# Attention: products of the identity in spare columns of two banks, at each step and around the first solve

## The chip, the cores and the metric

The kernel runs on one core of a Trainium2 chip. The metric is the device time of one execution in microseconds; the median of three runs of the kernel before is 908.11 us.

## The reference

Three parts follow each other. The change is in the first, a linear attention with a delta rule; for each of 4 x 8 heads, over 768 tokens and a head dimension of 48:

```python
k_n = k / (np.linalg.norm(k, axis=-1, keepdims=True) + 1e-06)
for t in range(S):
    y[:, :, t] = np.einsum('bhd,bhde->bhe', q[:, :, t], state)
    v_old = np.einsum('bhde,bhd->bhe', state, kt)
    state = state + bt[:, :, :, None] * np.einsum('bhd,bhe->bhde', kt, vt - v_old)
```

Its result goes through a mixer (real part of a two-dimensional Fourier transform, normalisation, two matrix products of width 1536) and a gated layer (products of width 1024 and one over the 768 tokens). Both are untouched.

## The kernel before

**Tiling.** The tokens are cut into chunks of 64. A group is 128 tokens of all heads; there are G = 6 groups. Each group has N = 8 steps, STEPS = 48 in all, and a step handles PR = 4 units (pairs of heads), one head on the lower 64 partitions and one on the upper 64. So nearly all products of this part are 64x64 or 64x48, in float32, and each one leaves two records in the trace.

**The solve.** Within a chunk the recurrence becomes a triangular system. VectorE inverts 32x32 blocks of one group at a time in `t_lane`, column by column: `column(g, j)` for j = 0 to H - 2 = 30, two operations each (L580, L584), and each raises the semaphore `chain` by one. Column j of group 0 is complete at `chain` = 2j + 4. Behind it `unlanes` transposes the result to `t_rows` (L591) and `t_cols` (L593). TensorE then couples the two blocks of a chunk: `couple_w` (L416, 32x32 products, called W below) and, from its copy `w_sb`, `couple_x` (L429, X below). ScalarE copies W and X out of PSUM and, with `corners` (L327), the inverses themselves, into `tt`. W and X of group 0 come before the loop; later groups' are spread over steps of the loop.

**The loop.** TensorE's order is written by hand, in `tensor(pe)`. At step k it does, in this order: the p products of step k (L455, into bank `ps_r`, from the state copy `s_sb` of four steps before), the u products of step k - 1 (L473, into `ps_u`, from `tt` and `r_sb`), at the first step of a group X, then the y products of step k - 2 (L490 and L495, into `ps_y`), the s products of step k - 2 (L508, into `ps_s`), and at some steps a piece of a later group's gram or score matrix (L404, into `ps_ga`) or W or X. ScalarE copies each bank to SBUF behind it (`r_sb` L351, `u_sb` L355, `s_sb` L367, `y_sb` L372) and raises `r_ok`, `u_ok`, `s_ok`, `y_ok`. `ps_u` is one bank and `ps_y` two banks of 512 columns; the u products use columns 0 to 191 of `ps_u`, the y products columns 0 to 191 of both banks of `ps_y`. `ident` is a 128x128 identity that GpSimd makes at the start; it is used for one product of 128x192 (L447).

**Before the loop** TensorE does 20 pieces (L404), whose last one ends while the solve of group 0 is still going on, then W and X of group 0, then starts the loop.

SyncE loads the inputs and stores the results, with waits on these semaphores; the change does not touch it. Nor does it touch ScalarE, VectorE or GpSimd.

Of the kernel before, what the change touches and what calls it, by code (L numbers as in the profile page):

```python
# [16 lines left out]
P = 128  # L17

def attention(nc, sems, kq_g, k_g, v_g, beta_g, x_scr):  # L20
# [9 lines left out]
    G, _, UD = k_g.shape  # L30
    D = 48
    U = UD // D
    C = 64
    H = 32
    N = 8
    NB = 4
    PR = U // N
# [29 lines left out]
    with ExitStack() as ctx:  # L67
# [27 lines left out]
        ident = sb("ident", [P, P])  # L95
# [17 lines left out]
        ps_r, ps_u = bank("ps_r"), bank("ps_u")  # L113
        ps_y = bank("ps_y", 2)
# [14 lines left out]
        chain = sem("chain")  # L129
# [261 lines left out]
        def tensor(pe):  # L391
# [4 lines left out]
            def piece(what, g, p):  # L396
                m = turn[what, g, p]
                bank_free(m)
                if p % 2 == 0:
                    pe.wait_ge(kq_in[g % 4][0 if what == "g" else 1][p // 2], 16 * (g // 4) + 16)  # L400
                for j in range(QU):
                    for lo in HEADS:
                        x = kq[g % 4][lo:lo + C, :, QU * p + j]
                        last = pe.matmul(ps_ga[m % 2][lo:lo + C, C * j:C * j + C], x[:, 0],  # L404
                                         x[:, 0 if what == "g" else 1], start=True, stop=True)
                last.then_inc(ga_done, 1)
# [13 lines left out]
            def couple_x(g, c):  # L420
# [9 lines left out]
                                         start=True, stop=True)  # L430
                last.then_inc(ga_done, 1)

            for what, g in FIRST:
                for p in range(4):
                    piece(what, g, p)
            couple_w(0, 0)
            couple_w(0, 1)
            couple_x(0, 0)
            couple_x(0, 1)
            pe.wait_ge(ident_ok, 2)  # L440
            for k in range(STEPS + 2):
                i, n = k // N, k % N
                if NB <= k < STEPS:
                    b = k % NB
                    if k == NB:
                        pe.wait_ge(v_ok, 1)
                        pe.matmul(ps_r[:, 0:PR * D], ident[:], v_in[i % 2][:, units(n)].rearrange("p u d -> p (u d)"),  # L447
                                  start=True, stop=False, skip_group_check=True)
                    else:
                        pe.wait_ge(preset_ok, k - NB)  # L450
                    pe.wait_ge(s_ok, k - NB + 1)
                    for j in range(PR):
                        for lo in HEADS:
                            rows = slice(lo, lo + C)
                            last = pe.matmul(ps_r[lo:lo + C, D * j:D * j + D], kq[i % 4][rows, 0, PR * n + j],  # L455
                                             s_sb[rows, b, j], start=False, stop=True, skip_group_check=True)
                    last.then_inc(p_done, 1)
                if 1 <= k <= STEPS:
                    j0 = k - 1
                    g, m, c = j0 // N, j0 % N, (j0 // NB) % 2  # L460
                    if m % NB == 0:
                        pe.wait_ge(corner_ok, 2 * (g + 1))
                        pe.wait_ge(ga_out, turn["x", g, c] + 1)
                        pe.wait_ge(v_ok, g + 1)
                    if j0 >= NB:
                        pe.wait_ge(r_ok, p_count(j0))
                    if j0 >= 1:
                        pe.wait_ge(u_ok, j0)
                    for j in range(PR):
                        for lo in HEADS:  # L470
                            rows = slice(lo, lo + C)
                            right = r_sb[rows, j0 % 2, j] if j0 >= NB else v_in[0][rows, PR * m + j]
                            last = pe.matmul(ps_u[lo:lo + C, D * j:D * j + D], tt[g % 2][rows, PR * m + j], right,  # L473
                                             start=True, stop=True)
                    last.then_inc(u_done, 1)
                if 0 < i < G and n == 0:
                    couple_x(i, 0)
                if k >= 2:
                    j0 = k - 2
                    g, m, b, c = j0 // N, j0 % N, j0 % NB, (j0 // NB) % 2  # L480
                    out = rows_of(g, c)
                    if j0 >= 1:
                        pe.wait_ge(y_ok, j0)
                    pe.wait_ge(u_ok, j0 + 1)
                    pe.wait_ge(masked, j0 // 2 + 1)
                    for j in range(PR):
                        for lo in HEADS:
                            at = 512 * (lo // C) + D * j
                            if j0 >= NB:
                                pe.matmul(ps_y[out, at:at + D], kq[g % 4][lo:lo + C, 1, PR * m + j],  # L490
                                          s_sb[lo:lo + C, b, j], start=True, stop=False)
                        for lo in HEADS:
                            at = 512 * (lo // C) + D * j
                            rows = slice(lo, lo + C)
                            last = pe.matmul(ps_y[out, at:at + D], score[g % 2][rows, PR * m + j],  # L495
                                             u_sb[rows, j0 % 2, j], start=j0 < NB, stop=True)
                    last.then_inc(y_done, 1)
                    if j0 < STEPS - NB:
                        if j0 == 0:
                            pe.wait_ge(s_zero, 2)  # L500
                        if j0 >= 2:
                            pe.wait_ge(s_ok, j0 - 1)
                        if m == 0:
                            pe.wait_ge(k_ld[g % 2], 16 * (g // 2) + 16)
                        for j in range(PR):
                            for lo in HEADS:
                                rows = slice(lo, lo + C)
                                last = pe.matmul(state(b, slice(lo, lo + D))[:, j], k_in[g % 2][rows, PR * m + j],  # L508
                                                 u_sb[rows, j0 % 2, j], start=False, stop=True,
                                                 skip_group_check=True)  # L510
                        last.then_inc(s_done, 1)
                if k >= STEPS:
                    continue
                if i and 2 <= n < 6 and i + 1 < G:
                    piece("a", i + 1, n - 2)
                if n >= 4 and i + 3 < G:
                    piece("g", i + 3, n - 4)
                if i and n == 1:
                    couple_w(i, 1)
                if i and n == 2:  # L520
                    couple_x(i, 1)
                if n == N - 1 and i + 1 < G:
                    couple_w(i + 1, 0)
# [1367 lines left out]
```

## Time and profile before

| | |
|---|---|
| median of three runs | 908.11 us (908.05 to 908.37) |
| the profiled execution | 913.28 us, span 911.5 us |
| TensorE busy | 837.3 us, 92% |
| VectorE, ScalarE, GpSimd busy | 477.4, 301.5, 199.2 us |
| mean granted clock of TensorE | 0.927 |
| attention's recurrence (first u product to the last y product) | 58.1 to 277.4 us |

### The profile page before, as it was taken

To read this page: it belongs to the slowest core of one execution; us is meant where nothing else is said; L and a number is where in the kernel's file an instruction comes from. 1 tells how busy PE (TensorE), PEld (TensorE's weight loads), DVE (VectorE), ACT (ScalarE), POOL (GpSimd) and SP (SyncE) were. 2 spreads that over 40 slices of the span, in tenths; PEclk is the share of its full clock that TensorE was granted. 3 is DMA by queue.
4 is the path that set the end of the run, shared out by engine and by line. 5 is a ranking of instruction groups with operands and counts; after the bars stand their busy time and mean duration, and the time that the engine had idled before them with its cause. 6 is when DMAs were issued, how large, how long until landed. Compare 5 with 4: busy or idle time off the path is not lost.

```text
span 911.5 us, 24639 instructions
## 1 busy us (share of the span) xinstructions
PE 837.3 (92%) x10634; PEld 811.5 (89%) x10634; DVE 477.4 (52%) x1092; ACT 301.5 (33%) x654; POOL 199.2 (22%) x167
## 2 busy tenths in 40 slices
PE   6378889899986799999999999999999999999998
PEld 6268888898885799999999999999889999899898
DVE  5999987979465574424442543433542432432421
ACT  4147374656532212211111211123441331331422
POOL 3123122031200530800270010000132222132231
PEclk9657787987978799999999999999999999999999
DMA  9600506134145121022000201201510010000001
GB/s 362 164 37 23 202 30 196 37 106 140 64 160 165 53 63 59 18 70 69 17 9 9 69 17 49 78 16 64 194 53 27 26 52 26 26 0 26 27 1 53
DMA packets 32889, 65.13 MB, mean 71 GB/s; under 512 B 3673, under 2 KB 25506, under 8 KB 32802
## 3 DMA queue, kind: packets, MB, share of 16 engines
q1 hardware_dynamic: 32802, 63.85, 20.8%
q8 instruction: 69, 1.13, 0.5%
q14 instruction: 18, 0.15, 0.1%
HBM read 46.86 MB, written 14.16 MB: 67 GB/s over the span
## 4 chain that ended last, share of the span: by engine, by line
PE 60%; issue 21%; DVE 11%; ACT 4%; POOL 2%; DMA 1%; SPq 1%; POOLq 0%; ACTq 0%; DVEq 0%
PE m_ps_h L1090 12%; PE g_ps_v L1601 11%; PE m_ps_d L1090 10%; PE ps_ga L404 4%; PE g_ps_y L1601 3%; PE ps_y L495 3%; PE ps_y L490 3%; DVE t_lane L584 2%; DVE prod L580 2%; PE ps_u L473 2%; PE ps_r L455 2%; POOL g_vn_lo L1498 2%; PE g_ps_u L1601 2%; PE ps_s L508 2%; ACT tt L327 2%
## 5 line engine op out<-in xcount | busy, mean ns | idle before, releaser
L1090 PE MATMUL m_ps_h<-m_unt_hi,m_w_hi 128*128 128x256 f32 x432 | 122.3, 283 | 2.8 <-DVE m_unt_lo L1280 2.1
L1090 PE MATMUL m_ps_h<-m_unt_lo,m_w_hi 128*128 128x256 f32 x432 | 121.4, 281 | 0.0
L1090 PE MATMUL m_ps_h<-m_unt_hi,m_w_lo 128*128 128x256 f32 x432 | 121.4, 281 | 0.0
L1286 DVE SCALAR_TENSOR_TENSOR m_h_lo<-m_ps_h,m_h_hi 128x512 fp32r<-128x512 f32 x72 | 49.8, 692 | 107.0 <-ACT m_h_hi L990 107.0
L1090 PE MATMUL m_ps_d<-m_w_hi,m_h_hi 128*128 128x384 f32 x288 | 97.6, 339 | 0.0
L1090 PE MATMUL m_ps_d<-m_w_hi,m_h_lo 128*128 128x384 f32 x288 | 96.4, 335 | 0.0
L1090 PE MATMUL m_ps_d<-m_w_lo,m_h_hi 128*128 128x384 f32 x288 | 96.3, 334 | 0.0
L990 ACT ACTIVATE m_h_hi<-m_ps_h 128x512 fp32r<-128x512 f32 x72 | 43.1, 598 | 150.8 <-PE m_ps_h L1090 150.8
L1090 PEld LDWEIGHTS m_ps_h<-m_unt_hi,m_w_hi 128*128 128x128 f32 x432 | 82.0, 190 | 3.4 <-DVE m_unt_lo L1280 2.5
L1090 PEld LDWEIGHTS m_ps_h<-m_unt_hi,m_w_lo 128*128 128x128 f32 x432 | 83.1, 192 | 0.0
L1090 PEld LDWEIGHTS m_ps_h<-m_unt_lo,m_w_hi 128*128 128x128 f32 x432 | 82.1, 190 | 0.0
L404 PE MATMUL ps_ga<-kq 64*64 64x64 f32 x1536 | 61.0, 236 | 13.8 <-issue 7.7
L584 DVE TENSOR_TENSOR t_lane<-t_lane,prod 128x31 f32<-128x31 f32 (+15 forms) x186 | 68.8, 370 | 6.4
L404 PEld LDWEIGHTS ps_ga<-kq 64*64 64x64 f32 x1536 | 57.3, 151 | 14.7 <-issue 8.3
L580 DVE TENSOR_TENSOR prod<-g_lane,t_lane 128x31 f32<-128x31 f32 (+15 forms) x186 | 63.7, 343 | 6.2
L1762 DVE TENSOR_TENSOR g_vs<-g_ps_v,g_bias 128x384 f32<-128x384 f32 x32 | 17.9, 558 | 92.3 <-PE g_ps_v L1601 92.0
L1498 POOL TENSOR_TENSOR g_vn_lo<-g_vn,g_vn_hi 128x512 fp32r<-128x512 f32 x24 | 30.5, 1286 | 161.5 <-ACT g_vn_hi L1540 161.5
L495 PE MATMUL ps_y<-u_sb,score 64*64 64x48 f32 x768 | 62.9, 248 | 2.2 <-issue 2.2
L490 PE MATMUL ps_y<-s_sb,kq 64*64 64x48 f32 x704 | 60.1, 247 | 4.8 <-issue 3.9
L1601 PE MATMUL g_ps_v<-g_ws_hi,g_vn_hi 128*128 128x384 f32 x192 | 64.4, 335 | 0.0
L1601 PE MATMUL g_ps_v<-g_ws_hi,g_vn_lo 128*128 128x384 f32 x192 | 64.1, 334 | 0.0
L1601 PE MATMUL g_ps_v<-g_ws_lo,g_vn_hi 128*128 128x384 f32 x192 | 64.1, 334 | 0.0
(220 smaller groups left out, 1947.6 us busy)
## 6 DMA issues: line engine op xcount, KB each, us to landing
kq<-kq_g SPq DMA_DIRECT2D x24, 512.0 KB, 7.0
v_in<-v_g SPq DMA_DIRECT2D x6, 768.0 KB, 8.7
k_in<-k_g SPq DMA_DIRECT2D x6, 768.0 KB, 10.6
x_scr<-y_sb SPq DMA_DIRECT2D x24, 192.0 KB, 1.9
stage<-w_ch SPq DMA_DIRECT2D x6, 768.0 KB, 8.7
x_scr<-m_x_sb SPq DMA_DIRECT2D x24, 192.0 KB, 1.9
g_x<-x_scr SPq DMA_DIRECT2D x24, 192.0 KB, 4.4
out<-g_y SPq DMA_DIRECT2D x24, 192.0 KB, 1.9
```

The source lines that it names most:

```text
L327: last = act.activation(tt[g % 2][quarter(a), :, H * (a % 2):H * (a % 2) + H], t_cols[quarter(a)], ACT.Copy)
L404: last = pe.matmul(ps_ga[m % 2][lo:lo + C, C * j:C * j + C], x[:, 0], x[:, 0 if what == "g" else 1], start=True, stop=True)
L455: last = pe.matmul(ps_r[lo:lo + C, D * j:D * j + D], kq[i % 4][rows, 0, PR * n + j], s_sb[rows, b, j], start=False, stop=True, skip_group_ ...
L490: pe.matmul(ps_y[out, at:at + D], kq[g % 4][lo:lo + C, 1, PR * m + j], s_sb[lo:lo + C, b, j], start=True, stop=False)
L495: last = pe.matmul(ps_y[out, at:at + D], score[g % 2][rows, PR * m + j], u_sb[rows, j0 % 2, j], start=j0 < NB, stop=True)
L580: dve.tensor_tensor(x, g_lane[g % 2][:, j + 1:H, j].unsqueeze(2).broadcast_to([P, m, n]), t_lane[:, j, 0:n].unsqueeze(1).broadcast_to([P, ...
L584: dve.tensor_tensor(below, below, x, ALU.add).then_inc(chain, 1)
L990: act.activation(h_hi[:, 2 * g:2 * g + 2], ps_h[g % 2][:, :].rearrange("p (f t) -> p f t", f=2), ACT.Relu).then_inc(h_hi_ok, 1)
L1090: last = pe.matmul(out, first[x], second[y], start=(k == 0 and m == 0), stop=(k == n - 1 and m == 2))
L1286: dve.scalar_tensor_tensor(h_lo[:, 2 * g:2 * g + 2].rearrange("p f t -> p (f t)"), ps_h[g % 2][:, :], 0.0, h_hi[:, 2 * g:2 * g + 2].rearra ...
L1498: pool.tensor_tensor(vn_lo[:, t], vn[:, t % 2], vn_hi[:, t].bitcast(F32), ALU.subtract).then_inc(vn_lo_ok, 1)
L1601: last = pe.matmul(out, first[x], second[w], start=(k == 0 and m == 0), stop=(k == n - 1 and m == 2))
```

## The change

A helper `keep_clock(ps, first)` issues one product with the identity as both operands, the second read as its first 64 columns repeated, into columns `first` to 511 of a bank. Nobody reads these columns. With `first` at its default they are columns 192 to 511, 320 of them, which no other product uses; with 0 it is the whole bank, 512 columns.

- Before W of group 0: nine products of 512 columns into `ps_u`, each behind a wait for one column of the solve (columns 22 to 30), then four without a wait. The wait for `ident_ok` is moved ahead of them.
- Between W and X three, and after X six more, of 512 columns.
- In the loop, ahead of the u products of each step (48 times) one of 320 columns into `ps_u`. The wait for `u_ok` is moved ahead of it and ahead of the waits for `corner_ok`, `ga_out`, `v_ok` and `r_ok`.
- Ahead of the y products of each step (48 times) one of 320 columns into `ps_y`, behind the wait for `y_ok` and ahead of the waits for `u_ok` and `masked`.

```diff
--- before.py
+++ after.py
@@ -430,14 +430,28 @@
                                          start=True, stop=True)
                 last.then_inc(ga_done, 1)
 
+            def keep_clock(ps, first=PR * D):
+
+                pe.matmul(ps[:, first:512], ident[:], ident[:, 0:C].unsqueeze(1).broadcast_to([P, (512 - first) // C, C]),
+                          start=True, stop=True)
+
             for what, g in FIRST:
                 for p in range(4):
                     piece(what, g, p)
+            pe.wait_ge(ident_ok, 2)
+            for j in range(H - 10, H - 1):
+                pe.wait_ge(chain, 2 * j + 4)
+                keep_clock(ps_u, 0)
+            for _ in range(4):
+                keep_clock(ps_u, 0)
             couple_w(0, 0)
             couple_w(0, 1)
+            for _ in range(3):
+                keep_clock(ps_u, 0)
             couple_x(0, 0)
             couple_x(0, 1)
-            pe.wait_ge(ident_ok, 2)
+            for _ in range(6):
+                keep_clock(ps_u, 0)
             for k in range(STEPS + 2):
                 i, n = k // N, k % N
                 if NB <= k < STEPS:
@@ -458,14 +472,15 @@
                 if 1 <= k <= STEPS:
                     j0 = k - 1
                     g, m, c = j0 // N, j0 % N, (j0 // NB) % 2
+                    if j0 >= 1:
+                        pe.wait_ge(u_ok, j0)
+                    keep_clock(ps_u)
                     if m % NB == 0:
                         pe.wait_ge(corner_ok, 2 * (g + 1))
                         pe.wait_ge(ga_out, turn["x", g, c] + 1)
                         pe.wait_ge(v_ok, g + 1)
                     if j0 >= NB:
                         pe.wait_ge(r_ok, p_count(j0))
-                    if j0 >= 1:
-                        pe.wait_ge(u_ok, j0)
                     for j in range(PR):
                         for lo in HEADS:
                             rows = slice(lo, lo + C)
@@ -481,6 +496,7 @@
                     out = rows_of(g, c)
                     if j0 >= 1:
                         pe.wait_ge(y_ok, j0)
+                    keep_clock(ps_y)
                     pe.wait_ge(u_ok, j0 + 1)
                     pe.wait_ge(masked, j0 // 2 + 1)
                     for j in range(PR):
```

TensorE's order around the first solve, before. W is L416, X is L429, and L473 are the first u products:

```order
L404 MATMUL ps_ga<-kq 64x64 x15
L416 MATMUL ps_ga<-t_rows,gram_sb 32x32 [waits trows_ok,ga_out]
L416 MATMUL ps_ga<-t_rows,gram_sb 32x32 x31
L416 MATMUL ps_ga<-t_rows,gram_sb 32x32 [waits trows_ok,ga_out]
L416 MATMUL ps_ga<-t_rows,gram_sb 32x32 x31
L429 MATMUL ps_ga<-t_cols,w_sb 32x32 [waits ga_out,tcols_ok]
L429 MATMUL ps_ga<-t_cols,w_sb 32x32 x31
```

The same place in the changed kernel, up to the first u products (L488 now):

```order
L435 MATMUL ps_u<-ident 128x512 [waits chain,ident_ok]
L435 MATMUL ps_u<-ident 128x512 [waits chain] x8
L435 MATMUL ps_u<-ident 128x512 x4
L416 MATMUL ps_ga<-t_rows,gram_sb 32x32 [waits trows_ok,ga_out]
L416 MATMUL ps_ga<-t_rows,gram_sb 32x32 x31
...
L435 MATMUL ps_u<-ident 128x512 x3
L429 MATMUL ps_ga<-t_cols,w_sb 32x32 [waits ga_out,tcols_ok]
L429 MATMUL ps_ga<-t_cols,w_sb 32x32 x31
...
L435 MATMUL ps_u<-ident 128x512 x6
L435 MATMUL ps_u<-ident 128x320
L488 MATMUL ps_u<-v_in,tt 64x48 [waits v_ok,ga_out,corner_ok]
```

Thirteen products of 512 columns now stand in front of W, three in front of X and six behind it.

TensorE's order in a step of the loop, before: p, u, y and s products with the waits that each carries:

```order
L455 MATMUL ps_r<-s_sb,kq 64x48 [waits s_ok,preset_ok]
L455 MATMUL ps_r<-s_sb,kq 64x48 x7
L473 MATMUL ps_u<-r_sb,tt 64x48 [waits u_ok,r_ok]
L473 MATMUL ps_u<-r_sb,tt 64x48 x7
L429 MATMUL ps_ga<-t_cols,w_sb 32x32 [waits ga_out,tcols_ok]
L429 MATMUL ps_ga<-t_cols,w_sb 32x32 x31
L490 MATMUL ps_y<-s_sb,kq 64x48 [waits masked,u_ok,y_ok]
```

The same step in the changed kernel:

```order
L469 MATMUL ps_r<-s_sb,kq 64x48 [waits s_ok,preset_ok]
L469 MATMUL ps_r<-s_sb,kq 64x48 x7
L435 MATMUL ps_u<-ident 128x320 [waits u_ok]
L488 MATMUL ps_u<-r_sb,tt 64x48 [waits r_ok]
L488 MATMUL ps_u<-r_sb,tt 64x48 x7
L429 MATMUL ps_ga<-t_cols,w_sb 32x32 [waits ga_out,tcols_ok]
L429 MATMUL ps_ga<-t_cols,w_sb 32x32 x31
L435 MATMUL ps_y<-ident 128x320 [waits y_ok]
L506 MATMUL ps_y<-s_sb,kq 64x48 [waits masked,u_ok]
```

The waits for `u_ok` and `y_ok` have moved to the new products; the others stay with the old ones.

## Rows read from the trace of the kernel before

**Rows 1.** The page: busy time by engine, and the granted clock in 40 slices

```profile
PE 837.3 (92%) x10634; PEld 811.5 (89%) x10634; DVE 477.4 (52%) x1092; ACT 301.5 (33%) x654; POOL 199.2 (22%) x167
PEclk9657787987978799999999999999999999999999
```

**Rows 2.** Stretches from group to group: length, busy time (count), clock, DMA

```profile
core 0: us, PE busy (x) PEld busy (x) DVE busy (x) ACT busy (x) POOL busy (x), PEclk, DMA share, GB/s
58.10:81.30 23.20, 20.57 (x533) 19.66 (x535) 21.59 (x50) 11.24 (x32) 4.97 (x3) 0.76 0.06 20
81.30:124.50 43.20, 39.86 (x1155) 38.86 (x1156) 39.37 (x93) 24.56 (x58) 12.44 (x10) 0.76 0.34 114
124.50:168.40 43.90, 38.98 (x1153) 37.55 (x1152) 36.58 (x86) 25.39 (x59) 8.77 (x6) 0.81 0.36 117
168.40:203.80 35.40, 31.98 (x1028) 30.87 (x1028) 29.30 (x63) 22.81 (x55) 8.71 (x6) 0.86 0.27 86
203.80:240.20 36.40, 33.82 (x1025) 32.65 (x1024) 30.63 (x67) 22.85 (x54) 9.24 (x6) 0.81 0.33 111
240.20:277.40 37.20, 31.77 (x948) 30.58 (x944) 17.45 (x24) 13.89 (x42) 0.50 (x2) 0.82 0.37 129
```

**Rows 3.** TensorE's waits in 58.1 to 277.4: who waited for whom, us, times, longest

```profile
PE ps_u L473 <- ACT tt L327: 7.0, 3, 4.1
PE ps_y L490 <- issue: 3.9, 3, 2.1
...
PE ps_ga L416 <- DVE t_rows L591: 2.2, 1, 2.2
...
PE ps_y L490 <- ACT y_sb L372: 0.8, 2, 0.6
```

**Rows 4.** TensorE's order of time, steps at both clocks: start, length, what

```profile
192.36 0.20 PE L455 MATMUL ps_r<-s_sb,kq 64*64 64x48 f32 x1
...
195.52 0.20 PE L455 MATMUL ps_r<-s_sb,kq 64*64 64x48 f32 x1
...
237.78 0.22 PE L455 MATMUL ps_r<-s_sb,kq 64*64 64x48 f32 x1
...
240.21 0.98 PE L416 MATMUL ps_ga<-t_rows,gram_sb 32*32 32x32 f32 x50
...
265.38 0.30 PE L455 MATMUL ps_r<-s_sb,kq 64*64 64x48 f32 x1
...
269.43 0.30 PE L455 MATMUL ps_r<-s_sb,kq 64*64 64x48 f32 x1
```

**Rows 5.** Order of time at 238 us: ScalarE's y copy, TensorE's y products

```profile
238.27 0.47 ACT L372 ACTIVATE y_sb<-ps_y 64x384 f32<-64x384 f32 x1
238.79 0.32 PE L490 MATMUL ps_y<-s_sb,kq 64*64 64x48 f32 x4
```

**Rows 6.** Order of time: 128-row float32 products, in the mixer and in the loop

```profile
284.57 2.78 PE L1054 MATMUL m_ps_h<-m_ts_sb,m_x_sin 128*96 128x193 f32 x16
...
64.64 1.01 PE L447 MATMUL ps_r<-v_in,ident 128*128 128x192 f32 x2
65.57 1.09 PE L455 MATMUL ps_r<-s_sb,kq 64*64 64x48 f32 x16
```

**Rows 7.** TensorE's order of time around the first solve; idle before, releaser

```profile
47.16 3.46 PE L416 MATMUL ps_ga<-t_rows,gram_sb 32*32 32x32 f32 x122 [10.73 <-DVE t_rows L591]
...
58.09 1.09 PE L473 MATMUL ps_u<-v_in,tt 64*64 64x48 f32 x16 [4.07 <-ACT tt L327]
```

**Rows 8.** VectorE's order of time: the second operations of columns 22 and 25

```profile
36.62 0.38 DVE L584 TENSOR_TENSOR t_lane<-t_lane,prod 128x207 f32<-128x207 f32 x1
...
41.78 0.32 DVE L584 TENSOR_TENSOR t_lane<-t_lane,prod 128x156 f32<-128x156 f32 x1
```

**Rows 9.** Stretches, columns as in rows 2: dense products at the mixer's start

```profile
303.70:308.00 4.30, 4.22 (x20) 4.22 (x21) 0.02 (x1) 0.00 (x0) 1.00 (x3) 0.50 0.05 20
308.00:312.00 4.00, 4.00 (x36) 4.00 (x36) 1.38 (x2) 2.57 (x3) 4.00 (x2) 0.98 0.00 0
```

## The prediction

> **What bounds the kernel now.** I read the page first, then a table of stretches cut where one group of the recurrence hands over to the next, then TensorE's order of time inside them. The page [rows 1] says TensorE is busy 92% of a span of 911.5 us, and its line of granted clock shows the only weak part: slices 2 to 14 stand between 5 and 9 tenths, everything later at 9. The later part (600 us of mixer and gated layer) holds neither of the banks that the change writes, so it can only start earlier or later. All is decided before 277.4 us.
>
> The table of stretches [rows 2] gives what I need. Group 0 of the recurrence runs from 58.1 to 81.3, groups 1 to 5 up to 277.4: 219.3 us. In each the granted clock is a mean of 1.0 (the 2.4 GHz level) and 0.5 (1.2 GHz), so a stretch of length T at mean c has 2(1-c)T at the low level: 11.1, 20.7, 16.7, 9.9, 13.8 and 13.4 us, **85.7 us** together. A kept clock can win only on these. TensorE is the bound in these stretches: TensorE's waits in the view of waits come to 22 us, eleven rows of which [rows 3] shows four (the 4.1 us of the first wait for tt lie ahead of 58.1 and are left out), and the DVE chain that solves the next group is ahead: the only wait for it inside is the 2.2 us at 81.
>
> **What a low clock costs here.** Two steps of the loop without a gram or score piece: from the first p product to the next step's first product it is 237.78 to 240.21 = 2.43 us at the high level and 265.38 to 269.43 = 4.05 us at the low one [rows 4]. So time at the low level would shrink by 1 - 2.43/4.05 = 40%. A step with a piece takes 195.52 - 192.36 = 3.16 us at the high level [rows 4]; its products stand without a gap, the other has one: y at 238.79 waits for the ACT copy of the y before it, 238.27 + 0.47 [rows 5]. Without that gap of some 0.2 us the share would be 45%. I take 43%: 85.7 x 0.43 = **37 us won**, if the clock stays up throughout.
>
> **What the fillers cost.** There is one of 128x320 ahead of each of the 48 u products and one ahead of each of the 48 y products: 96. They stand in TensorE's own order, and the steps have no hole there, so each is added whole, unless a wait stood behind it. The trace has no such product. From below: the mixer's products with 193 columns, 128 rows and a loaded weight for each follow each other 2.78 us for 16 records, (2.78 - 0.33)/15 = 0.163 us a record, two records a product, which is two clocks per column and record, with the weight load entirely beneath [rows 6]. So 320 columns are 2 x 320 x 2/2400 = 0.53 us at least: 51 us for 96. From above: the one product of the identity that stands among the small ones, 128x192 at the low clock, takes from 64.64 to the next at 65.57 = 0.93 us [rows 6], of which 0.64 are its columns and 0.29 loads that nothing covers; halved for the high clock, 0.53 + 0.145 = 0.68 us: 65 us for 96. I take 0.60 us, between them, since the loads' uncovered part is seen only once and beside a first use of v_in: 96 x 0.60 = **57.6 us lost**.
>
> **What the fillers hide.** A filler is free where TensorE would have waited. In [rows 3]: tt 2.9 (without the 4.1), t_rows 2.2, y_sb 0.8, and two smaller rows of ScalarE's 0.7, together 6.6 us, all of which come from other engines that go on while TensorE multiplies; I count them as gone. Waits without a releaser ("issue") are six rows, 3.9 the largest, 15.4 us in sum; I read them as instructions that arrive late, and since a filler gives their supply 0.6 us more I count half, 7.7 us. The gap for y_ok of [rows 5], about 0.2 us in the 20 of 48 steps without a piece, is behind the u filler too: 4 us. Together **18.3 us**. The moved wait for u_ok costs nothing: it asks for the copy of the step before, which stands on ScalarE ahead of the y copy at 238.27 [rows 5], and that one is not waited for in a step with a piece. Queued behind it are only products that wait for the same or more.
>
> **The first solve.** Before, W starts at 47.16 and takes 3.4 us, X ends at 54.0, and u starts at 58.09 after 4.07 us of waiting for tt [rows 7]. After, nine fillers of 128x512 follow the columns 22 to 30 and four more come behind them. Column 22 ends at 37.0 and 25 at 42.1 [rows 8]; the later ones take less than a filler each. At 512 columns a filler is 1.7 us at the low clock and 0.87 at the high one (the same arithmetic). The clock is taken as low when they start, for TensorE idles 10.7 us here in the trace of before [rows 7]. How fast dense products bring it back: from 303.7 to 308.0 the granted clock was 0.50 under 4.2 us of them, from 308 to 312 it was 0.98 [rows 9]. So three fillers run slow to 42, and ten more at 0.87 end at 50.8; W ends at 53.1 (2.3 us at the high clock instead of 3.4), three fillers 2.6, X 2.3, six fillers 5.2: 63.4. ScalarE needs 4.1 us behind X in the trace of before and X would end at 58.2, so it would be ready at about 62.3. u thus starts at 63.4 instead of 58.1: **5.3 us lost**. Nothing catches this up: the wait of 2.2 us at 81 is in the 18.3 already.
>
> **Sum.** + 57.6 + 5.3 - 37 - 18.3 = **+7.6 us**: a span of 919.1 instead of 911.5, and against the median of 908.1 (the profiled execution itself took 913.3) **915.7 us**.
>
> **Two rules of the Trainium skill.** The page "TensorE: Matmul & The Clock Gate" (Terms) puts the penalty of a throttled clock at the throttled time times (1 - K/N), here one half. An estimate by it would be 85.7 x 0.5 = 42.9 us won, and the sum +1.7 us; the rows of the two steps disagree, since small products do not shrink by half. The same page (Part 2, step-by-step) says that a weight load is pulled ahead of products in flight when row groups do not conflict or when it goes to the background weight buffer. By that rule the 0.29 us at 64.64 would not recur and a filler would cost 0.53 us; this is the price in the first rival.
>
> **The rivals.** *Not slower: the fillers are cheap and fill real holes.* Each costs its columns, 51 us in place of 57.6; all 15.4 us of issue waits go, not half; the low clock was worth 43 us. Then 51 + 5.3 - 43 - (6.6 + 15.4 + 4) = -12.7 us, 895 us; with the first two alone about -6.7 us, 901 us. Place: every step. It decides from the point where fillers plus first phase (56 to 63 us) cost less than clock and holes give back. For it: the mixer's steady row [rows 6]. Against it: only 22 us of waits stand against 96 fillers, and a piece step has none. Chance 0.24.
>
> *The clock is not kept.* If the clock falls because of the waits of 1 to 2.7 us [rows 3] and of the small products around them, and fillers keep it up in half of the places only, 18 us of gain are missing and the fillers in them cost double, some 20 x 0.6 = 12 us more: +38 us, 946 us. Against it: dense products of 128 rows brought the clock back [rows 9], and every step now holds over 1 us of them. That the change does nothing for the clock at all would be worse still and is in this case. Chance 0.12.
>
> *Nearly even.* A filler of 0.56 us and issue waits that go by two thirds: 57.6 - 3.8 and 18.3 + 2.6 give about +1. This lies between forecast and first rival. Chance 0.07. *The forecast*, slower by 2 to 20 us: 0.57.
>
> **How the numbers follow.** Bounds of the unknown costs: fillers -6.6 to +7.4 us, issue waits -7.7 to +7.7, clock -6 to +3. The range takes the forecast's and the nearer part of both rivals: 900 to 930 us; left out are the far end of the first rival (0.08) and the lost clock (0.12). A difference of 0.2%, 1.8 us, is about what a measurement can tell from none. Faster 0.24, within it 0.07, slower 0.69.
>
> **What the profile of the changed kernel would show.** Granted clock near 1.0 in all stretches from 58 to the end of the recurrence; groups 1 and 2 of nearly the old length (43 us), groups 3 and 4 some 2 to 3 us longer than 35.4 and 36.4; steps with a piece of 4.4 us instead of 3.16; u first at 63, not 58; TensorE's idle in the recurrence down from 22 to about 8 us. I would be wrong by the filler's price if two fillers lengthen the 3.16 us step by less than 1.1 us; by the clock, if a stretch below 0.9 is left; by the first phase, if ACT and not TensorE is last at 63; and by the rest, if the mixer and the gated layer (634 us from 277.4 on) change their length.

## The result

The changed kernel takes 953.1 us (median of 4 runs, 951.16 to 956.59) against 908.24 us of the kernel before: a ratio of 1.0495, with a 95% interval of 1.0461 to 1.0528. That is 44.9 us slower. The forecast was 7.6 us slower, 915.7 us, with a range to 930: the direction is right, the size is wrong by a factor of six. The profiled executions are 951.16 and 913.28 us; their spans, 949.2 and 911.5 us, differ by 37.7 us, and this part can be followed in the traces. Where the executions of one kernel lie more than 1.5% apart (e4 below, alone), its time and ratio are those of the faster ones, as the others were in a slower state.

The page of the changed kernel, engines and granted clock, answers to [rows 1]:

```profile
PE 901.7 (95%) x10870; PEld 818.9 (86%) x10870; DVE 475.9 (50%) x1092; ACT 301.3 (32%) x654; POOL 200.4 (21%) x167
PEclk9899899999999869999999999999999999999999
```

Nearly all slices of the recurrence now stand at 9, where [rows 1] had 5 to 8. TensorE is busy for 64 us more. The table of stretches answers to [rows 2]: six groups of the recurrence from 64.0 to 315.2, columns as there, and two stretches for the rest of the kernel:

```profile
64.00:90.50 26.50, 26.07 (x543) 19.34 (x543) 21.45 (x49) 10.07 (x30) 8.72 (x6) 1.00 0.03 11
90.50:141.50 51.00, 47.28 (x1192) 37.72 (x1189) 37.24 (x92) 25.20 (x60) 8.72 (x6) 0.93 0.31 101
141.50:187.80 46.30, 44.63 (x1194) 36.06 (x1191) 35.91 (x83) 25.25 (x60) 9.79 (x6) 1.00 0.33 111
187.80:230.00 42.20, 40.56 (x1054) 32.12 (x1052) 33.55 (x73) 23.52 (x56) 8.72 (x6) 1.00 0.23 72
230.00:271.40 41.40, 40.70 (x1068) 32.26 (x1064) 23.64 (x50) 22.55 (x54) 9.19 (x6) 1.00 0.29 98
271.40:315.20 43.80, 41.88 (x1007) 31.90 (x1003) 22.53 (x34) 13.88 (x41) 0.50 (x2) 1.00 0.32 115
315.20:348.00 32.80, 19.27 (x102) 17.67 (x101) 15.18 (x39) 6.71 (x12) 6.08 (x7) 0.64 0.40 128
348.00:949.00 601.00, 592.57 (x3814) 577.00 (x3813) 236.74 (x556) 150.82 (x309) 132.49 (x109) 1.00 0.13 42
```

The recurrence takes 251.2 us instead of 219.3, it starts later by 6, and what follows it is unchanged (949.2 - 315.2 = 634.0 us, before 911.5 - 277.4 = 634.1). So every group is slower than before, although five of the six have the full clock. Only the second stretch has time at the low clock, some 7 us by 2(1-c)T, behind a wait of 3 us that begins at 109.

TensorE's waits from 64.0 to 315.2 (who waited for whom, us in total, times, longest) answer to [rows 3]:

```profile
PE ps_ga L429 <- issue: 3.0, 1, 3.0
PE ps_u L488 <- ACT tt L327: 1.8, 4, 0.5
PE ps_y L506 <- issue: 1.8, 2, 1.3
PE ps_y L435 <- ACT y_sb L372: 1.2, 4, 0.6
PE ps_r L469 <- issue: 1.0, 1, 1.0
```

These are the five largest of eight rows; all of them together are 10.0 us, where they were 22. The wait for `u_ok`, moved ahead of the filler, shows as 0.4 us behind ScalarE's copy of `u_sb`, as much as in the kernel before: moving it cost nothing that shows. And one step with a piece, TensorE's order of time, answers to the first two of [rows 4]:

```profile
217.56 0.20 PE L469 MATMUL ps_r<-s_sb,kq 64*64 64x48 f32 x1
...
218.24 0.81 PE L435 MATMUL ps_u<-ident 128*128 128x320 f32 x2
218.97 0.67 PE L488 MATMUL ps_u<-r_sb,tt 64*64 64x48 f32 x16
219.57 0.81 PE L435 MATMUL ps_y<-ident 128*128 128x320 f32 x2
220.31 0.32 PE L506 MATMUL ps_y<-s_sb,kq 64*64 64x48 f32 x4
...
222.45 0.20 PE L469 MATMUL ps_r<-s_sb,kq 64*64 64x48 f32 x1
```

The step is 222.45 - 217.56 = 4.89 us, where it was 3.16, both at the high clock and without a wait. Two fillers cost 1.73 us, 0.865 each; forecast were 0.60. From the start of a filler to the start of the next product it is 0.73 us. The other 0.13 us stand ahead of it: p, 0.54 us from its first product to the first u product in a step of before (192.36 to 192.90), now takes 0.68 until the filler starts. Nine steps, with and without a piece, are at the high clock and without a wait in both traces; they grew by 1.66 to 1.78 us, 1.73 in the mean. The first u product of the step of before:

```profile
192.90 0.50 PE L473 MATMUL ps_u<-r_sb,tt 64*64 64x48 f32 x11
```

### The profile page after: what moved, and what is told of

It is laid out like the page before. It is cut to its first block, busy times and chain, and to the rows that moved or that the text cites. A ratio compares the mean times of both kernels' runs of the same rounds, so it can differ in the third digit from the quotient of the medians.

```text
span 949.2 us, 25078 instructions
## 1 busy us (share of the span) xinstructions
PE 901.7 (95%) x10870; PEld 818.9 (86%) x10870; DVE 475.9 (50%) x1092; ACT 301.3 (32%) x654; POOL 200.4 (21%) x167
## 4 chain that ended last, share of the span: by engine, by line
PE 67%; issue 19%; DVE 6%; ACT 4%; POOL 2%; DMA 1%; SPq 1%; POOLq 0%; ACTq 0%; DVEq 0%
PE m_ps_h L1106 12%; PE g_ps_v L1617 11%; PE m_ps_d L1106 10%; PE ps_u L435 5%; PE ps_ga L404 4%; PE ps_y L435 4%; PE g_ps_y L1617 3%; PE ps_u L488 3%; PE g_ps_u L1617 3%; PE ps_y L506 3%; PE ps_y L511 2%; PE ps_r L469 2%; ACT tt L327 2%; POOL g_vn_lo L1514 2%; PE ps_s L524 1%
## 5 line engine op out<-in xcount | busy, mean ns | idle before, releaser
L596 DVE TENSOR_TENSOR prod<-g_lane,t_lane 128x31 f32<-128x31 f32 (+15 forms) x186 | 70.6, 380 | 6.2
L600 DVE TENSOR_TENSOR t_lane<-t_lane,prod 128x31 f32<-128x31 f32 (+15 forms) x186 | 66.2, 356 | 6.4
L404 PE MATMUL ps_ga<-kq 64*64 64x64 f32 x1536 | 55.0, 224 | 14.2 <-issue 8.5
L404 PEld LDWEIGHTS ps_ga<-kq 64*64 64x64 f32 x1536 | 51.6, 139 | 15.0 <-issue 9.1
L1617 PE MATMUL g_ps_v<-g_ws_hi,g_vn_hi 128*128 128x384 f32 x192 | 64.4, 335 | 0.0
L435 PE MATMUL ps_u<-ident 128*128 128x320 f32 (+1 forms) x140 | 61.4, 546 | 1.5 <-DVE t_lane L600 1.0
L1520 POOL TENSOR_TENSOR g_g<-g_vs,g_ut 128x384 f32<-128x384 f32 x32 | 36.8, 1149 | 113.9 <-DVE g_vs L1778 113.9
```

Source lines behind the costliest of these rows:

```text
L435: pe.matmul(ps[:, first:512], ident[:], ident[:, 0:C].unsqueeze(1).broadcast_to([P, (512 - first) // C, C]), start=True, stop=True)
L596: dve.tensor_tensor(x, g_lane[g % 2][:, j + 1:H, j].unsqueeze(2).broadcast_to([P, m, n]), t_lane[:, j, 0:n].unsqueeze(1).broadcast_to([P, ...
L600: dve.tensor_tensor(below, below, x, ALU.add).then_inc(chain, 1)
L1520: pool.tensor_tensor(g[:, n % 2], vs[:, n % 2], ut[:, f, HS * h:HS * h + HS], ALU.mult).then_inc(g_ok, 1)
L1617: last = pe.matmul(out, first[x], second[w], start=(k == 0 and m == 0), stop=(k == n - 1 and m == 2))
```

## The experiments

Short diffs are against the changed kernel, if nothing else is said. All but the changed kernel itself ran beside the kernel before at 911.4 to 912.3 us, so that ratios are given and not only times. "Low" is the time at the low clock in the recurrence, worked out as in the prediction, 2(1-c)T, from a row of the table of stretches. It is that of the one execution in the profile. A filler is said to cost what a step with a piece grows by; the step of before taken for this is the one of 3.16 us.

**e1_first_only.** The 22 products around the first solve alone.

```diff
-                    keep_clock(ps_u)
...
-                    keep_clock(ps_y)
```

> Only the 22 products of 512 columns around the first solve stand; the loop has none and its waits are where they were after the change. In the changed kernel the first u product starts at 64.7 us instead of 58.1. Theory A (the first phase is worth its own delay): the loop starts some 6 us late, runs group 0 at the high clock where it ran 11 us at the low one (about 5 us back), and the wait for t_rows at 81 (2.2 us) takes up the rest: 907 to 910 us, with the low clock back from group 1 on. Theory B (the delay goes through to the end): 914 us. Neither gives a part of the 45 us worth naming; above 920 us both are wrong.

915.6 us against 911.4, ratio 1.0046 (1.0022 to 1.0071): 4 us slower than its own run of before, between the 1 us less to 2 us more of theory A and the 6 us more of theory B. In its trace the first u product stands at 64.4 (58.1 before) and the last y product ends at 277.6 (277.4 before): there the delay is caught up, as theory A has it, with a granted clock of 0.97 from 64.4 to 86. The span is 912.0 against 911.5 us. The medians show 4 us more than the traces do; what they are is open. In either case the first phase is not where 45 us went.

**e2_loop_only.** The 96 products in the loop alone; the fillers before W, between W and X and behind X are taken out.

```diff
-            for j in range(H - 10, H - 1):
-                pe.wait_ge(chain, 2 * j + 4)
-                keep_clock(ps_u, 0)
-            for _ in range(4):
-                keep_clock(ps_u, 0)
...
-            for _ in range(3):
-                keep_clock(ps_u, 0)
...
-            for _ in range(6):
-                keep_clock(ps_u, 0)
```

> Only the 96 products of 320 columns in the loop stand, none around the first solve. Theory A (the fillers in the loop carry the loss, at 0.87 us each instead of the 0.60 forecast): 943 to 949 us, steps with a piece of 4.9 us as in the changed kernel. Theory B (a good part of the 45 us is the first phase): 930 us or less.

953.7 us, ratio 1.0459 (1.0427 to 1.0490). Relative to its own run of before that is 42.3 us slower, of the 44.9 us of the whole change. The time lies above theory A's 949, as the kernel before stood 3 us higher beside it than in the runs from which 949 was made. Steps with a piece like the one above take 4.89 to 4.91 us. The loss is in the loop.

**e3_loop_u_only.** Of e2, the fillers ahead of u alone.

```diff
-                    keep_clock(ps_y)
```

> Only the 48 products of 320 columns ahead of the u products stand. Against the run with both, 48 fillers fewer. Theory A (0.87 us each: 0.53 of columns, 0.2 of weight loads that nothing covers, 0.15 because neighbours no longer overlap): 42 us less than with both, if one per step keeps the clock: 902 to 908 us, steps with a piece 4.0 us. Theory B (0.60 us each, the rest of the loss lies elsewhere in the loop, in the moved waits or in the supply of instructions): 29 us less, 915 to 919 us. If one per step doesn't keep the clock, the granted clock falls below 0.9 in some group and the time lies 10 to 25 us above either.

921.3 us, ratio 1.0110 (1.0079 to 1.0141), 32.5 us less than e2. A step with a piece, TensorE's order of time:

```profile
199.54 0.20 PE L460 MATMUL ps_r<-s_sb,kq 64*64 64x48 f32 x1
...
200.22 0.81 PE L435 MATMUL ps_u<-ident 128*128 128x320 f32 x2
200.96 0.49 PE L479 MATMUL ps_u<-r_sb,tt 64*64 64x48 f32 x10
...
203.57 0.20 PE L460 MATMUL ps_r<-s_sb,kq 64*64 64x48 f32 x1
```

4.03 us, 0.87 more than without a filler: theory A's price, and not B's. The time by itself would not tell: it is 32.5 us less than e2, nearer to the 29 of theory B than to the 42 of A. What is missing to A's 902 to 908 is the clock, the third case of the expectation: one filler per step keeps it less well. Its recurrence:

```profile
57.70:284.40 226.70, 209.79 (x5920) 180.34 (x5920) 179.54 (x387) 121.32 (x299) 45.65 (x32) 0.93 0.30 100
```

Low are 2 x 0.07 x 226.7 = 32 us, where e2 has 26 and the changed kernel 5 to 7. TensorE also waits more, 18.5 us in the recurrence against 13.8 in e2.

**e4_loop_64cols.** Of e2, with fillers of 64 columns.

```diff
-                    keep_clock(ps_u)
+                    keep_clock(ps_u, 448)
...
-                    keep_clock(ps_y)
+                    keep_clock(ps_y, 448)
```

> All 96 fillers of the loop, each of 64 columns instead of 320; none around the first solve. The 256 columns less are 2 x 256 x 2/2400 = 0.43 us each. Theory A (a fixed part of 0.34 us each beside the columns): 0.44 to 0.5 us each, 36 to 41 us less than with 320 columns: 903 to 912 us if the clock stays up. Theory B (the price is columns alone): 0.11 us each and some 70 us less, 875 us. If such short fillers don't keep the clock, the granted clock of the groups is near that of before (0.76 to 0.86) and the time is above 925 us by A.

943.1 us, the median of its two faster executions (936.8 and 949.5), ratio 1.0348 (1.0259 to 1.0437); the other two took 958.4 and 961.5 us, and the profile is of the longest. Its recurrence:

```profile
58.10:324.90 266.80, 251.32 (x6017) 233.05 (x6018) 181.04 (x391) 121.05 (x299) 45.11 (x32) 0.78 0.26 85
```

Low are 2 x 0.22 x 266.8 = 117 us, more than the 86 to 88 of the kernel before. But this is the slowest execution: its mean granted clock over the whole span is 0.916, and that of the two faster ones is 0.928 and 0.938, where the kernel before beside it had 0.923 to 0.938. So these fillers left the clock about as it was without any. A step with a piece at the high clock:

```profile
216.91 0.20 PE L460 MATMUL ps_r<-s_sb,kq 64*64 64x48 f32 x1
...
217.59 0.43 PE L435 MATMUL ps_u<-ident 128*128 128x64 f32 x2
...
218.56 0.43 PE L435 MATMUL ps_y<-ident 128*128 128x64 f32 x2
...
221.06 0.20 PE L460 MATMUL ps_r<-s_sb,kq 64*64 64x48 f32 x1
```

4.15 us: 0.50 us for each filler of 64 columns, of which the columns would be 0.11. The fixed part is there, 0.39 us where it is 0.34 with 320 columns, so theory A holds for the price, and the last case of the expectation for the clock (above 925 us).

**f2_u_twice.** Of e3, with two fillers in a row.

```diff
                     keep_clock(ps_u)
+                    keep_clock(ps_u)
```

> As the run with fillers ahead of the u products alone (e3), with two of 320 columns in a row in each place. Step with a piece 3.16 us without, 4.03 with one. Theory A (what a filler costs beyond its columns comes from the change between it and small neighbours: an uncovered weight load, and neighbours that drain): the second one costs its columns alone, 0.53 us, step 4.56 us, 25 us more than e3, 943 to 948 us. Theory B (each product of 128 rows costs 0.87 us wherever it stands): step 4.90 us, 42 us more, 960 to 965 us.

935.0 us, ratio 1.0246 (1.0223 to 1.0268).

```profile
208.65 0.20 PE L460 MATMUL ps_r<-s_sb,kq 64*64 64x48 f32 x1
...
209.33 1.34 PE L435 MATMUL ps_u<-ident 128*128 128x320 f32 x4
...
213.22 0.20 PE L460 MATMUL ps_r<-s_sb,kq 64*64 64x48 f32 x1
```

4.57 us: the second filler costs 0.54 us, which is its columns (0.53) and nothing else. Theory A. It holds 96 fillers as e2 does, and is 18.7 us faster than e2, of which 48 x (0.87 - 0.54) = 16 us are the fixed part paid once per step and not twice. It stayed under the expected 943 us. Part of that is the clock: low are 2 x 0.04 x 246.0 = 20 us, 12 fewer than in e3, worth 5 us by the prediction's 43%; the waits fell by 4 us (18.5 to 14.7); the rest of the 12 us to e3's 921.3 + 48 x 0.54 = 947.2 is not accounted for.

**f3_u_32weights.** Of e3, with the first 32 columns of the identity as weights.

```diff
-                pe.matmul(ps[:, first:512], ident[:], ident[:, 0:C].unsqueeze(1).broadcast_to([P, (512 - first) // C, C]),
+                pe.matmul(ps[0:32, first:512], ident[:, 0:32], ident[:, 0:C].unsqueeze(1).broadcast_to([P, (512 - first) // C, C]),
```

> As e3, but the weights of the filler are the first 32 columns of the identity, not all 128, and it writes 32 partitions; rows and moving columns are the same. Theory A1 (the fixed part of 0.34 us is mostly the load of 128 weight columns): a filler costs 0.65 to 0.7 us, step with a piece 3.8 to 3.9 us, 8 to 10 us less than e3, 910 to 913 us if the clock is kept as in e3. Theory A2 (the fixed part is the drain of neighbours): step 4.0 us, time as e3. If a quarter of the columns doesn't keep the clock, the mean granted clock falls from 0.957 towards 0.93.

918.3 us, ratio 1.0093 (1.0061 to 1.0124), 3 us less than e3. A step with a piece, 197.60 to 201.55, is 3.95 us, 0.08 less than e3's:

```profile
197.60 0.20 PE L460 MATMUL ps_r<-s_sb,kq 64*64 64x48 f32 x1
...
198.28 0.73 PE L435 MATMUL ps_u<-ident 128*32 128x320 f32 x2
198.94 0.49 PE L479 MATMUL ps_u<-r_sb,tt 64*64 64x48 f32 x10
...
201.55 0.20 PE L460 MATMUL ps_r<-s_sb,kq 64*64 64x48 f32 x1
```

Three quarters of the weight load gone are worth 0.08 us, in this step and in most others, all of it behind the filler: from its start to the next product it is 0.66 us, 0.74 in e3, while the 0.68 us ahead of it stay. So an estimate is that about 0.1 of the fixed 0.34 us is the load; the rest must come from the neighbours, nearer to A2. Low are 2 x 0.05 x 223.4 = 22 us; over whole executions the mean granted clock is that of e3 (0.954 to 0.965, e3 0.954 to 0.963).

**f5_u_64rows.** Of e3, with 64 rows and 64 weight columns.

```diff
-                pe.matmul(ps[:, first:512], ident[:], ident[:, 0:C].unsqueeze(1).broadcast_to([P, (512 - first) // C, C]),
+                pe.matmul(ps[0:C, first:512], ident[0:C, 0:C], ident[0:C, 0:C].unsqueeze(1).broadcast_to([C, (512 - first) // C, C]),
```

> As e3, but the filler uses 64 rows and 64 weight columns of the identity, 320 moving columns: a quarter of the array. Theory A (small neighbours overlap with it as with each other, at least those on the other 64 rows): a filler costs 0.55 to 0.7 us, step with a piece 3.7 to 3.85 us. Theory B (a product as long as this holds up all that follows): step 4.0 us as in e3. Clock: if what counts is that TensorE multiplies at all, mean clock as in e3 (0.957); if it is how much of the array works, it is nearer to that of before (0.927). Time 905 to 925 us.

919.5 us, ratio 1.0087 (1.0053 to 1.0121). TensorE's order of time:

```profile
199.56 0.20 PE L460 MATMUL ps_r<-s_sb,kq 64*64 64x48 f32 x1
...
200.01 0.45 PE L435 MATMUL ps_u<-ident 64*64 64x320 f32 x1
...
200.07 0.28 PE L479 MATMUL ps_u<-r_sb,tt 64*64 64x48 f32 x2
200.30 0.43 PE L435 MATMUL ps_u<-ident 64*64 64x320 f32 x1
...
203.06 0.20 PE L460 MATMUL ps_r<-s_sb,kq 64*64 64x48 f32 x1
```

The step is 3.50 us: the filler costs 0.34 us, less than its own columns (0.53). Set step by step against the kernel before, where both are at the high clock and without a wait (eight steps), it costs 0.34 to 0.70 us, 0.50 in the mean; against the same steps of e3 it is cheaper in every one, by 0.2 to 0.55 us. Products of p and u stand between and beside its two records, as at 200.07. This is the other half of the proof. It differs from e3's filler in rows and in weight columns, and f3, with fewer weight columns still but all rows, costs 0.79; so what made a filler dear is that it takes all 128 rows, and nothing runs beside it. It also writes the same bank, `ps_u`, so the bank is not what is dear. But it does not do the work it is there for:

```profile
58.10:284.10 226.00, 210.92 (x5920) 192.19 (x5920) 179.04 (x384) 121.06 (x299) 45.65 (x32) 0.84 0.30 100
```

Low are 72 us, where e3, with as many columns on all rows, has 32, and f3, with all rows and 32 weight columns, 22. Over whole executions the mean granted clock is 0.931 to 0.940, below all of e3 and f3.

**f4_edges.** Of e3, in the first three steps of groups 1 to 5 alone. These are 16 fillers and not the 15 expected: the edit's condition also holds at step 48, behind the last group.

```diff
-                    keep_clock(ps_u)
+                    if k >= N and n < 3:
+                        keep_clock(ps_u)
```

> As e3, but the filler ahead of the u products stands only in the first three steps of groups 1 to 5 (15 in all), where the wait for tt, W and X are and no piece stands, and where the clock fell in the trace of before. Theory A (a filler costs 0.87 us, and the clock falls at the edges): 13 us lost of which some 3 lie in waits, and up to 37 us won: 895 to 903 us if 15 hold the clock through the edges; 908 to 915 us if the clock still falls at half of the edges. Theory B (the clock needs a filler at every step): mean granted clock as before, 0.927, and 918 us or more.

914.2 us, ratio 1.0020 (1.0001 to 1.0039): theory A's second case, in which the clock still falls at half of the edges. Low are 2 x 0.14 x 221.0 = 62 us.

**g1_edges_dense.** Of e3, with two, three and one fillers in those steps, 30, and two more at step 48: 32 in all.

```diff
-                    keep_clock(ps_u)
+                    for _ in range((2, 3, 1)[n] if k >= N and n < 3 else 0):
+                        keep_clock(ps_u)
```

> No fillers around the first solve and none ahead of y. Ahead of the u products of groups 1 to 5 stand two fillers of 320 columns in the group's first step, three in the second (the one that waits for tt), one in the third: 30 in all. By the prices measured so far (0.87 us for the first of a row, 0.54 for each further one) they cost 5 x (3 x 0.87 + 3 x 0.54) = 21 us, of which some 7 lie in the waits for tt. With one per step at the edges (15) the clock still fell at four of five edges. Theory A (more of them in a row carry the clock through the edges): granted clock of 58 to 300 us at 0.93 or more, up to 30 us won, 900 to 906 us. Theory B (the falls have nothing to do with how dense the edge is): clock as with 15, 0.85, fillers at the low clock at twice the price, 920 us or more.

915.9 us, ratio 1.0052 (1.0031 to 1.0073): neither. Low fell to 2 x 0.09 x 220.6 = 40 us, so the clock went most of theory A's way, yet the recurrence takes 220.6 us, 1.3 more than before. Its waits without a releaser are 20.3 us, in the kernel before 15.4; the largest rows of its waits:

```profile
PE ps_s L515 <- issue: 6.7, 3, 3.1
PE ps_u L480 <- issue: 4.1, 2, 3.5
PE ps_u L480 <- ACT tt L327: 4.0, 1, 4.0
PE ps_ga L429 <- issue: 3.5, 2, 3.3
PE ps_ga L404 <- issue: 3.0, 2, 2.3
```

48 us less at the low clock are 21 us by the prediction's 43%, the fillers cost 23 (those 21 and 1.4 at step 48), and the waits without a releaser take 5 more. Why they grow was not tried.

**g2_loop_y_only.** The other half of e2: the fillers ahead of y alone.

```diff
-                    keep_clock(ps_u)
```

> The other half of e3: only the 48 fillers ahead of the y products. Theory A (0.87 us each, in whichever place): step with a piece 4.0 us, time within 4 us of e3, 917 to 925 us. Theory B (one of the two places is the dear one, the moved wait for y_ok holding up the y products): step with a piece above 4.2 us and 930 us or more, and e3 owes its better time to the place.

935.0 us, ratio 1.0248 (1.0218 to 1.0277), 13.8 us above e3. Theory B's time, but not its reason: steps with a piece like e3's take 4.03 us, the same 0.87 us a filler. The clock is what differs:

```profile
58.10:305.60 247.50, 233.32 (x5923) 199.73 (x5924) 178.71 (x388) 120.25 (x299) 46.08 (x32) 0.83 0.27 92
```

Low are 84 us against e3's 32. In each group the step that waits for tt has nothing of 128 rows between its p products and the wait here. One of these waits is 2.11 us at 188.7, and the clock is low from about 193 to 203:

```profile
190.80 0.67 PE L478 MATMUL ps_u<-r_sb,tt 64*64 64x48 f32 x16 [2.11 <-ACT tt L327]
```

52 us more at the low clock than in e3 are 22 us by the 43%. That is too much for the 13.8 us of the medians, since the profile is of the longest of its five executions, 941.5 us, with a mean granted clock of 0.931; the other four had 0.942 to 0.947 and e3's 0.954 to 0.963. So the clock is worse in all of them, though by less than the two traces say. Why the place decides was not isolated.

**g3_no_piece.** Of e3, in the 20 steps of groups 1 to 5 that hold no piece, and, by the same condition, at step 48: 21 fillers.

```diff
-                    keep_clock(ps_u)
+                    if i and not (2 <= n < 6 and i + 1 < G or n >= 4 and i + 3 < G):
+                        keep_clock(ps_u)
```

> One filler of 320 columns ahead of the u products in those 20 steps of groups 1 to 5 that hold no piece (the pieces, 64x64 products in a row, brought the clock back in the trace of before). Theory A (a filler only where the step has nothing dense keeps the clock as one per step does): 17 us lost instead of 42, clock 0.92 in 58 to 300 us, 898 to 906 us. Theory B (the clock then falls in the edges as with 15 there): clock 0.85, 913 to 920 us.

917.2 us, ratio 1.0048 (1.0028 to 1.0069): nearer to theory B, with a granted clock of 0.87 from 58 to 300 us (low 54 us in its recurrence).

**g4_short_first.** Of g1, with a first phase of five fillers behind columns 26 to 30 and two behind X.

```diff
-            for j in range(H - 10, H - 1):
+            for j in range(H - 6, H - 1):
...
-            for _ in range(4):
-                keep_clock(ps_u, 0)
...
-            for _ in range(3):
-                keep_clock(ps_u, 0)
...
-            for _ in range(6):
+            for _ in range(2):
```

> As g1_edges_dense, with a shorter first phase: five products of 512 columns behind columns 26 to 30 of the solve and two behind X (the changed kernel has 9 + 4, 3 and 6). They end before W's inputs are there but for some 2 us. Theory A (what is kept from the change's first phase is the high clock of W, X and group 0, some 5 us at a cost of 3): within 3 us of g1_edges_dense, first u product at 58 to 60 us. Theory B (fewer of them don't lift the clock): first u product at 60 us or later with a granted clock of 0.5 in group 0, 3 to 6 us above g1_edges_dense.

917.6 us, ratio 1.0067 (1.0033 to 1.0101), first u product at 59.9: within 2 us of g1, theory A as far as the scatter lets one say. None of the versions is faster than the kernel before.

## Why the prediction was wrong, step by step

**The filler's price.** This is the step that failed. The prediction took 0.60 us between 0.53 and 0.68; the trace shows 0.87 (e3, e2, g2 and the changed kernel alike). The upper bound was the one product of the identity in the trace, at 64.64, from its own start to the next one's.
**The clock.** Right. The low time went from 85.7 to some 7 us, worked out by stretches as there; none of the six groups is below 0.9, and the time left at the low clock is from about 111 to 118, at a wait of 3 us. The 43% agree with a step of before that has neither a piece nor a gap: 235.48 to 237.78 = 2.30 us at the high clock, against the 4.05 us at the low one, is a share of 43%.

**What the fillers hide.** The waits fell by 12.0 us (22.0 to 10.0), not by 14.3; of the issue waits 8.8 us went (15.4 to 6.6), as forecast 7.7, and the others fell by 3.2, not 6.6. The gap behind y_ok gave back less than forecast. Two steps in a row without a piece; the first starts in the kernel before with

```profile
235.48 0.20 PE L455 MATMUL ps_r<-s_sb,kq 64*64 64x48 f32 x1
```

and the second is that of [rows 4], 237.78 to 240.21. The same two in the changed kernel:

```profile
263.77 0.20 PE L469 MATMUL ps_r<-s_sb,kq 64*64 64x48 f32 x1
...
267.80 0.22 PE L469 MATMUL ps_r<-s_sb,kq 64*64 64x48 f32 x1
...
271.89 1.20 PE L416 MATMUL ps_ga<-t_rows,gram_sb 32*32 32x32 f32 x64
```

The first grew from 2.30 us (235.48 to 237.78) to 4.03, by 1.73 us, as a step with a piece does; the second, the one of the gap, from 2.43 (237.78 to 240.21) to 4.09, by 1.66. So the fillers hid 0.07 us there and not 0.2. The steps without a piece are also 24 of 48 and not 20 (20 in groups 1 to 5 and 4 in group 0). Together this is under 2 us, where 4 were forecast.

**The sum again**, with measured terms, for the recurrence: 96 x 0.87 = 83.5, less 0.43 x (85.7 - 7) = 34, less 8.8 and 3.2, less 0 to 2 for the gap, is + 36 to + 38 us. Measured are 251.2 - 219.3 = 31.9 us, so the sum is 4 to 6 us too high. The clock has two digits, and with the low times of the whole recurrence (87.7 and 5.0 us, from 0.80 and 0.99) it comes 2 us nearer; the rest is open. It is small against the 83.5 us of the fillers, and against the 26 us by which their price was wrong.

**The first phase.** Forecast +5.3 us with u at 63.4 (its terms add up to 63.2) and a filler of 0.6 ahead of it, so 64.0; measured 64.67. Thirteen fillers ended at 51.7 (50.8 forecast), W at 53.9 (53.1). TensorE, not ScalarE, was last, as said. Without the loop's fillers (e1) the trace shows almost no loss at the end, 0.2 us, and group 0 then runs at the high clock; in the sum of the prediction that gain stood under the clock. TensorE's order of time answers to [rows 7]:

```profile
37.65 14.14 PE L435 MATMUL ps_u<-ident 128*128 128x512 f32 x26 [1.05 <-DVE t_lane L600]
51.72 2.21 PE L416 MATMUL ps_ga<-t_rows,gram_sb 32*32 32x32 f32 x128
...
64.67 0.67 PE L488 MATMUL ps_u<-v_in,tt 64*64 64x48 f32 x16
```

**The groups.** Forecast were nearly the old lengths for groups 1 and 2 and 2 to 3 us more for 3 and 4. Measured are 51.0, 46.3, 42.2 and 41.4 us against 43.2, 43.9, 35.4 and 36.4.

**The two rules of the Trainium skill.** The penalty of a low clock as throttled time times one half ("TensorE: Matmul & The Clock Gate", Terms) gives 39 us for the clock in the sum above instead of 34, and the sum 30 to 32 us. The sum, 4 to 6 us off by itself, cannot decide between the two; the steps do, with 2.30 against 4.05 us. The rule that a weight load is pulled ahead of the products in flight when the row groups do not conflict or the background weight buffer takes it (same page, Part 2) agrees with the trace between two fillers, 0.54 us, and in the mixer [rows 6]; between a small product and a filler a load of about 0.1 us was left, estimated from f3, and the rule says nothing of the rest of the 0.34 us.

**The rivals.** The cheap filler fell with its price. The clock not kept did not come about in the changed kernel, but in part it did in five of its shorter versions (e4, f4, f5, g2, g3), with 54 us or more at the low clock in their profiles; none of them wins.

**What stays open.** The medians differ by 44.9 us, the profiled executions by 37.9; of the 37 us by which the medians miss the forecast, 7 are this. The profiled one of before is 5 us above its median and that of the changed kernel 2 below; the trace of a 908 us execution was not there to compare, and e1's 4 us may be of the same kind. The waits without a releaser vary from run to run of nearly the same program (6.6 to 20.3 us), and this may be part of it. Each kernel has one trace, so the times at the low clock are of one execution each.

## What to carry to other kernels

The price of an inserted instruction is the change in the distance between its neighbours' neighbours, not its own duration: among products that overlap on different rows, one that takes all rows costs its columns and 0.34 us here. Before paying for a clock, multiply: some 80 us fewer at the low clock gave about 34 us, and the waits gave 12, so 96 fillers could win only at under 0.5 us apiece, less than their columns alone take (0.53), and they cost 0.87. Those of 64 columns (0.50) or 64 rows (0.50 in the mean) were cheaper and did not keep the clock. If fillers must be, stand them together (the second one cost 0.54 us). Those ahead of u kept the clock better than those ahead of y; that this is because they stand ahead of the wait for `tt` was not tested.

## What the runs showed that was not expected

A filler on 64 rows and 64 weight columns, with the same 320 columns (f5), left the clock low for 72 us; one on 128 rows with 32 weight columns (f3) left it low for 22 us, like the full one with 32 us (e3). All executions agree: the mean granted clock over the whole span was 0.931 to 0.940 in f5, 0.954 to 0.965 in f3, 0.954 to 0.963 in e3, and 0.919 to 0.940 in the kernel before beside them. A filler of 128 rows and 64 columns twice a step (e4) left the clock where it was without any. And 48 fillers ahead of u kept it better than the same 48 ahead of y: 32 against 84 us in the profiles, with 13.8 us between the medians.
